# Two probability tiles per GpSimd subtraction, with a ring of four unsplit tiles, in an attention and feed-forward kernel

## What is computed

```python
q, k, v: (2, 8, 768, 64) fp32;  proj: (64, 6)
q_bucket, k_bucket = 6-bit hashes: signs of q @ proj and of k @ proj
scores = q @ k.T / 8, and -1e9 where q_bucket != k_bucket
attn = exp(scores - max(scores)); attn = attn / (sum(attn) + 1e-9)
x = (attn @ v), heads side by side: (1536, 512)
h = max(x @ w1, x @ w2, x @ w3)          # (1536, 768)
y = h @ w_out                            # (1536, 512)
out = elu(y @ w_in) @ w_out2             # (1536, 2048) -> (1536, 512)
```

## Time and profile before

| | |
|---|---|
| median of 3 runs | 778.21 us |
| lowest, highest | 777.1, 780.05 us |
| span of the profiled execution, first to last instruction | 777.8 us |
| TensorE busy | 745.1 us, 96% of the span |
| VectorE busy | 388.9 us, 50% |
| ScalarE busy | 396.5 us, 51% |
| GpSimd busy | 369.3 us, 47% |
| mean granted TensorE clock | 0.994 |

### The profile page before, as it was taken

How to read it: one execution, slowest core, us unless ns; L and a number is a source line. 1 busy time by engine, 2 the same in 40 slices (tenths; PEclk the granted TensorE clock), 3 DMA queues, 4 the chain that set the end, 5 groups by cost and what they waited for, 6 DMA issues and landing times.

```text
span 777.8 us, 11623 instructions
## 1 busy us (share of the span) xinstructions
PE 745.1 (96%) x3920; PEld 677.1 (87%) x3920; DVE 388.9 (50%) x616; ACT 396.5 (51%) x748; POOL 369.3 (47%) x294
## 2 busy tenths in 40 slices
PE   4699999989999998999999999999999999999997
PEld 3488888868888877999998998999999998998996
DVE  3677888877888874322214333333322214333333
ACT  1268879777887885222225444443322225444442
POOL 5177889877988997332123332331332123332330
PEclk9999999999999999999999999999999999999999
DMA  6756363562615300411122112122511122112112
GB/s 135 172 116 147 85 130 88 117 148 52 148 42 130 103 0 1 115 48 42 41 67 82 55 58 77 54 82 92 151 42 42 41 68 82 54 55 79 54 41 81
DMA packets 81515, 62.56 MB, mean 80 GB/s; under 512 B 28992, under 2 KB 72768, under 8 KB 81472
## 3 DMA queue, kind: packets, MB, share of 16 engines
q1 hardware_dynamic: 81472, 62.02, 30.6%
HBM read 38.81 MB, written 3.15 MB: 54 GB/s over the span
## 4 chain that ended last, share of the span: by engine, by line
PE 57%; ACT 1%; DVE 1%; DMA 0%; issue 0%; DVEq 0%
PE banks L677 14%; PE banks L679 14%; PE banks L678 13%; PE banks L1039 6%; PE banks L1040 6%; PE banks L1042 5%; DVE gl L973 0%; DVE g_sb L970 0%; DMA out_dram<-out_sb 0%; ACT neg L922 0%; ACT gh L924 0%; PE banks L1048 0%; ACT neg L920 0%; DVE out_sb L981 0%; ACT out_sb L931 0%
## 5 line engine op out<-in xcount | busy, mean ns | idle before, releaser
L868 POOL TENSOR_TENSOR wl<-raw,wh 128x1024 fp32r<-128x1024 f32 (+3 forms) x50 | 126.3, 2526 | 317.7 <-ACT wh L900 317.7
L331 POOL TENSOR_TENSOR p_lo<-probs,p_hi 128x384 fp32r<-128x384 f32 x192 | 200.1, 1061 | 64.8 <-ACT p_hi L379 63.9
L378 ACT ACTIVATE probs<-banks 128x384 f32<-128x384 f32 x192 | 94.9, 494 | 46.4 <-PE banks L606 44.0
L478 DVE TENSOR_REDUCE half_max<-banks 128x1 f32<-128x384 f32 x192 | 99.3, 547 | 34.3 <-PE banks L593 33.1
L677 PE MATMUL banks<-xh,wh 128*128 128x384 f32 x288 | 96.5, 335 | 0.4 <-PEq L126 0.3
L679 PE MATMUL banks<-xh,wl 128*128 128x384 f32 x288 | 96.2, 334 | 0.0
L678 PE MATMUL banks<-xl,wh 128*128 128x384 f32 x288 | 96.2, 334 | 0.0
L379 ACT ACTIVATE p_hi<-banks 128x384 fp32r<-128x384 f32 x192 | 94.4, 492 | 0.0
L964 DVE TENSOR_SCALAR g_sb<-banks 128x384 f32<-128x384 f32 x64 | 35.5, 557 | 116.6 <-ACT neg L920 116.6
L677 PE MATMUL banks<-yh,wh 128*128 128x384 f32 x256 | 86.0, 336 | 0.0
L679 PE MATMUL banks<-yh,wl 128*128 128x384 f32 x256 | 85.9, 336 | 0.0
(11 more groups left out here) (114 smaller groups left out, 1495.8 us busy)
## 6 DMA issues: line engine op xcount, KB each, us to landing
operands<-wh SPq DMA_DIRECT2D x36, 384.0 KB, 7.0
raw<-in_moe_w SPq DMA_DIRECT2D x36, 256.0 KB, 3.8
raw<-in_moe_w_in SPq DMA_DIRECT2D x32, 256.0 KB, 2.7
raw<-in_moe_w_out SPq DMA_DIRECT2D x32, 256.0 KB, 2.9
wl<-wh SPq DMA_DIRECT2D x12, 384.0 KB, 5.8
q_raw<-in_q SPq DMA_DIRECT2D x16, 192.0 KB, 3.5
k_raw<-in_k SPq DMA_DIRECT2D x16, 192.0 KB, 3.7
v_raw<-in_v SPq DMA_DIRECT2D x16, 192.0 KB, 2.4
```

The costliest lines, as they stand in the source:

```text
L331: pool.tensor_tensor(p_lo[:, at, :], probs[:, step % RING, :], p_hi[:, at, :].bitcast(FP32), ALU.subtract).then_inc(pl_done, 1)
L378: act.activation(probs[:, step % RING, :], scores, ACT.Exp, scale=SCALE)
L478: dve.tensor_reduce(half_max[:, m % 2, n // 2, n % 2:n % 2 + 1], mx_ps[n % 2][:, 0:HALF], AX.X, ALU.max).then_inc(mx_read, 1)
L868: pool.tensor_tensor(wl[:, j, 0:cols], raw[:, j, 0:cols], wh[:, j, 0:cols].bitcast(FP32), ALU.subtract).then_inc(w_ready, 1)
```

## The change

GpSimd no longer subtracts after every step, but after every odd step for the two tiles of that step and the one before: one operation of 128 partitions by 768 columns in place of two of 384. The `probs` ring grows from 3 tiles to 4 (PROBS = 4), so that a pair lies side by side. `pl_done` counts pairs now, 6 per head where it was 12. ScalarE waits for it only in even steps (for the pair of steps s-4 and s-3); TensorE's `weigh` waits for the pair that holds its tile.

```diff
 RING = 3
+PROBS = 4
...
-        probs = sb("probs", [P, RING, HALF])
+        probs = sb("probs", [P, PROBS, HALF])
...
                 for step in range(STEPS):
-                    if s.has_st:
+                    if s.has_st and step % 2 == 1:
                         pool.wait_ge(exp_done, s.count(STEPS, step + 1))
-                        at = (STEPS * s.off + step) % KEPT
-                        pool.tensor_tensor(p_lo[:, at, :], probs[:, step % RING, :], p_hi[:, at, :].bitcast(FP32),
-                                           ALU.subtract).then_inc(pl_done, 1)
+                        at, of = (STEPS * s.off + step - 1) % KEPT, (step - 1) % PROBS
+                        pool.tensor_tensor(p_lo[:, at:at + 2, :], probs[:, of:of + 2, :],
+                                           p_hi[:, at:at + 2, :].bitcast(FP32), ALU.subtract).then_inc(pl_done, 1)
...
                         wait(act, pv_step, s.count(STEPS, step + 1 - KEPT))
-                        wait(act, pl_done, s.count(STEPS, step + 1 - RING))
+                        if step % 2 == 0:
+                            wait(act, pl_done, s.count(T, (step - PROBS) // 2 + 1))
                         act.wait_ge(st_ready, s.count(STEPS, step + 1))
                         scores = st_ps[step % RING][:, 0:HALF]
-                        act.activation(probs[:, step % RING, :], scores, ACT.Exp, scale=SCALE)
+                        act.activation(probs[:, step % PROBS, :], scores, ACT.Exp, scale=SCALE)
...
-                pe.wait_ge(pl_done, s.count(STEPS, step - LAG + 1))
+                pe.wait_ge(pl_done, s.count(T, (step - LAG) // 2 + 1))
```

## The result

The changed kernel takes 787.11 us (median of 4 runs, 786.62 to 787.52) against 777.66 us before (now the median of 4 runs): ratio 1.0116, 95% interval 1.0096 to 1.0135. It is slower by 1.2%, inside the range, and beyond the 782.5 us forecast. The profiled execution has a span of 785.7 us, 7.9 more than the profiled one of the kernel before; between the medians lie 9.5. Sums of spans are therefore good to about 2 us.

A forecast was written before the change was run, and what follows sets the result against it. TensorE was taken to bound the kernel, leaning on VectorE. The terms, +5.0 for VectorE's waiting and -0.8 for the last head, put the 777.8 us span at 782.0; adjusted for the runs' median and clock, 782.5, range 775 to 790.

The forecast's parts named there:

- What bounds the kernel: Middle heads: TensorE busy 65.36 of 66 us, leaning on VectorE through the PSUM ring of two banks for the maxima.
- GpSimd's own time: `p_lo` subtractions: 200.1 us become 176.4, 23.7 less busy time, or 13 to 25; priced at nothing.
- rival 2: Faster, 773 us: `v_lo` and `empty` fall into GpSimd's longer free stretches in most heads; chance 0.11.
- When results come: Later `p_lo` pairs are covered, by 0.9 us on ScalarE and several on TensorE; 0 to 1 us in the middle heads.
- VectorE's waiting: `v_lo` and `empty` wait for GpSimd's longer operation in flight: 7.5 us more on VectorE.
- The walk through two slot ends: Four `v_lo` and `empty` operations followed singly: 3.65 us more in two heads, 29 us over 16; the upper end.
- the mean: Average rest of GpSimd's operation over all arrival times: 0.68 us against 0.44, so 7.5 us more over 32 operations.
- How much reaches TensorE: Two thirds of VectorE's 7.5 us of added waiting reach TensorE: +5.0 us.
- The waits of rows 3: TensorE's weight loads waited 9.4 us in 16 places, read as about one per head, margin near zero in half the cases.
- The last head: ScalarE's last exponential loses its 0.85 us wait for `p_lo`: 0.8 us back, between 0 and 0.9.
- The clock: Last head's granted clock of 0.92, against 1.00 in the middle heads, costs 1.7 us; no change counted.
- rival 3: Much slower, 792 us: 3 of 4 operations behind a fresh pair in every head, half of 29 us reaching TensorE; chance 0.12.

The follow-up runs named there:

- pair_standins: Changed kernel with VectorE's `v_lo` and `empty` replaced by reciprocals of 64 columns, so neither result is computed; 766.34 us.
- two_short: Changed kernel with each pair subtracted by two operations of 384 columns back to back, signalled after the second; 774.12 us.
- ring4_alone: Kernel before with only the `probs` ring grown to four tiles, still one subtraction of 384 columns per step; 771.54 us.
- before_eight_waits: Kernel before, ring of three, with eight long-fulfilled waits added on ScalarE in the first head; 781.28 us, ratio 1.0029 to before.
- ring4_halves: Kernel before with a `probs` ring of four and each tile subtracted in two operations of 192 columns; 807.87 us.
- ring4_v_gpsimd: Kernel before with a `probs` ring of four and `v_lo` subtracted by GpSimd in place of VectorE; 773.87 us.
- pair_ve_gpsimd: Changed kernel with `v_lo` and `empty` both computed by GpSimd in place of VectorE; 772.40 us.

## Why the prediction was right, and where its terms were off

The direction and the mechanism were right. That the time fell inside the range was luck in part: two errors of opposite sign met, as the last point shows.

- **What bounds the kernel.** Right: TensorE, leaning on VectorE through the two banks of the maxima. The loss in the regular heads shows in that wait.
- **GpSimd's own time.** 176.4 us were forecast, 180.2 measured: right in direction, worth nothing, as said. The lower end of the "13 to 25 us" beside it does not follow from the rows: by the median it would be 192 x 1.013 - 176.4 = 18.1 us, and the groups by shape show 19.9. That GpSimd's relief shows in the time somewhere (rival 2) has no row.
- **When results come.** Priced at 0 to 1 us. pair_standins and two_short bear it out for the middle heads. In one place, head 1 (60.11 us), ScalarE waited 2.01 us for a pair, against the sign that its waits would stay below 1 us. In two_short the wait was 1.75 us, in the last head.
- **VectorE's waiting.** The mechanism was right and the size half of what it was: 7.5 us forecast, 15.4 measured (47.2 us in all, beyond the 36 to 44 that were named as the sign). The walk through two slot ends named the single operations well. It gave 1.2, 2.25, 2.2 and 2.2 us for the four; in the changed trace the same four took 1.18, 2.24, 2.12 and 1.49. Three of four were right to 0.1 us. Carried over 16 heads it gave 29 us, twice too much, so neither the mean nor the walk had the size. The mean takes arrivals as random, but a hand-ordered slot repeats them: in heads 5, 7, 9 and 11 `v_lo` meets the start of a pair and takes 2.25 us, in 4, 6, 8, 10 and 12 it takes 1.48 to 1.49.
- **How much reaches TensorE.** Two thirds were taken, 5.0 us. The span of the changed kernel less that of two_short is 14.3 us, for 15.4 on VectorE, and less that of ring4_alone 14.2: more than nine tenths. The waits of rows 3 had been read as about one per head, and that was wrong. Of the 16 places five lie in head 0, and heads 2, 5, 7, 9 and 11 have none. Yet in 5, 7, 9 and 11 the `v_lo` that grew by 1.5 us makes the weight load wait 1.6 us, and the head is 1.6 us longer. So the margin was near zero also where no wait showed it.
- **The last head.** Right: 0.8 us back was forecast, and the last head went from 20.6 to 19.7. TensorE's wait there fell from 2.01 to 1.15 us, and ring4_alone has it at 1.17.

```profile
310.28 0.44 PE L622 MATMUL banks<-p_hi,v_hi 128*128 128x384 f32 x1 [1.15 <-ACT inv L358]
```

- **The clock.** The prediction put 1.7 us on the low clock of the last head and counted no change. before_eight_waits bears the size out: the same head and the same ring of three, with a wait of 1.99 us, took 19.1 us at a granted clock of 1.00 and 20.6 at 0.92. The mean granted clock differs between executions of one kernel too (ring4_alone: 0.983 to 0.998), one more reason not to read single spans to the microsecond.
- **Not in the sum at all: the loop's turn.** The kernel before stalls there, the changed one does not. By ring4_alone that is 5.3 us over heads 7 and 8 (4.4 and 0.9). The pair's cost of 14.2, less 0.9 for the last head and 5.3 for the turn, is 8.0, the 7.9 of the spans. So the forecast was 9.2 us short on the pair, and a gain of 5.3 us that it did not know of hid more than half of that. With the stall still there the changed kernel would have taken about 792 us (787.1 + 5.3, an estimate from these runs), outside the range of 775 to 790. That is the time of rival 3, whose price, half of 29 us, is close to the 14.2 that were measured. Without the stall in either kernel the change costs 1.8% (against two_short) to 2.2% (against ring4_alone).

## What to carry to other kernels

Before making GpSimd's operations longer, list what VectorE runs beside them of the two kinds that waited here: a subtraction of two SBUF tensors (`v_lo`) and a `tensor_scalar` from SBUF to SBUF (`empty`). Follow each through a few repetitions of the schedule: the wait is set by phase, not by an average, and may run through a whole train of GpSimd operations. Shorter operations of GpSimd are no sure remedy: from 768 to 384 columns gave 787.11 to 774.12 us, from 384 to 192 columns gave 771.54 to 807.87. Moving those few operations to ScalarE and GpSimd made the kernel 1.5% faster than before, where the change made it 1.2% slower. And when a small edit gives or takes half a per cent at one place, look at whether it is a loop's branch: one idle wait more on ScalarE was worth 0.9%.

## What the runs showed of the hardware

- VectorE can lose to GpSimd several times in a row: 5.29 us through nine operations of 0.6 to 1.0 us (ring4_halves), 4.38 us through four of about 1.0 (ring4_v_gpsimd).
- VectorE's reciprocal and reduction ran beside GpSimd without delay: 541 to 553 ns for 16 reciprocals of 64 columns (pair_standins), and 493 to 561 ns for the 192 maxima of 384 columns in the changed kernel, 494 to 559 before.
- GpSimd's subtraction or product takes 1.84 us for 768 columns on 128 partitions and 1.83 us on 12 (pair_ve_gpsimd).
- A loop's turn cost ScalarE 2.0 to 5.0 us that the profile puts on no other engine, or nothing, depending on one instruction far ahead of it. With the stall three or four packets moved on the instruction queue next to the branch, without it one or none.
- TensorE's granted clock over the head behind that stall was 0.76 to 0.96 in the five kernels with it and 1.00 in ring4_alone, two_short and the changed kernel, without it.
